# Attention and two expert layers on one core: what releases the loads of q, k and v

## The reference, cut to what matters

```python
scores = scale * np.matmul(q_c, k_c.transpose(0, 1, 2, 4, 3))   # chunks of 64
attn = softmax(scores)                                          # row max taken off, 1e-9 in the sum
out = np.matmul(attn, v_c)
```

## Time and profile before

| | |
|---|---|
| median of 3 runs | 1944.83 us |
| the profiled execution's own time | 1944.43 us |
| its span, first to last instruction | 1942.6 us |
| TensorE busy | 1926.2 us (99%) |
| VectorE, ScalarE, GpSimd busy | 1101.3, 721.2, 520.3 us |
| mean granted clock of TensorE | 1.000 |
| traffic of memory | 61.40 MB, mean 32 GB/s |

### The profile page before, as it was taken

One profiled execution on the slowest core, in us unless ns is written; L12 is line 12 of the kernel. 1 busy time (PEld: TensorE's weight loads), 2 busy tenths in 40 slices (PEclk: granted clock), 3 DMA queues, 4 the chain that ended last, 5 costly groups with the idle time before them and its releaser, 6 DMA issues.

```text
span 1942.6 us, 31606 instructions
## 1 busy us (share of the span) xinstructions
PE 1926.2 (99%) x10756; PEld 1733.7 (89%) x10756; DVE 1101.3 (57%) x1831; ACT 721.2 (37%) x1527; POOL 520.3 (27%) x592
## 2 busy tenths in 40 slices
PE   7999999999999999999999999999999999999999
PEld 6889999999999999999999999999999988888898
DVE  7846655455455555554555555545555586666666
ACT  6632332233223222223232222232332475555554
POOL 6522262222222222222222222222222362222220
PEclk9999999999999999999999999999999999999999
DMA  7100000000000000000000000000000000000002
GB/s 259 70 33 22 22 23 22 22 32 23 31 23 22 22 22 22 22 22 22 22 22 22 22 22 22 22 22 22 22 22 22 22 23 23 22 22 22 22 22 97
DMA packets 19626, 61.40 MB, mean 32 GB/s; under 512 B 2304, under 2 KB 2304, under 8 KB 19584
## 3 DMA queue, kind: packets, MB, share of 16 engines
q1 hardware_dynamic: 19584, 60.84, 9.2%
HBM read 56.12 MB, written 4.72 MB: 31 GB/s over the span
## 4 chain that ended last, share of the span: by engine, by line
PE 98%; DMA 1%; DVE 0%; issue 0%; ACT 0%; SPq 0%; ACTq 0%; DVEq 0%
PE up_banks L598 45%; PE mid_banks L615 4%; PE mid_banks L616 4%; PE mid_banks L628 4%; PE mid_banks L620 4%; PE mid_banks L629 4%; PE mid_banks L630 4%; PE last_banks L628 3%; PE last_banks L620 3%; PE last_banks L616 3%; PE last_banks L615 3%; PE last_banks L629 3%; PE last_banks L630 3%; PE bank L616 1%; PE bank L620 1%; PE bank L615 1%
## 5 line engine op out<-in xcount | busy, mean ns | idle before, releaser
L598 PE MATMUL up_banks<-x_hi,w_hi 128*128 128x384 f32 x1680 | 566.1, 337 | 0.3 <-ACT h_raw L1231 0.3
L598 PE MATMUL up_banks<-x_hi,w_lo 128*128 128x384 f32 x1680 | 564.9, 336 | 0.0
L598 PE MATMUL up_banks<-x_lo,w_hi 128*128 128x384 f32 x1680 | 563.2, 335 | 0.0
L1231 ACT ACTIVATE h_raw<-up_banks 128x384 f32<-128x384 f32 x360 | 176.4, 491 | 727.6 <-PE up_banks L598 717.3
L1654 DVE TENSOR_TENSOR h_raw<-up_banks,h_raw 128x384 f32<-128x384 f32 x360 | 200.4, 557 | 406.0 <-PE up_banks L598 404.2
L414 POOL TENSOR_TENSOR w_sum<-raw 128x256 f32<-128x256 f32 x80 | 59.5, 744 | 1165.9 <-PE up_banks L598 1159.0
L598 PEld LDWEIGHTS up_banks<-x_hi,w_hi 128*128 128x128 f32 x1680 | 315.4, 188 | 10.7 <-ACT h_raw L1231 0.7
L598 PEld LDWEIGHTS up_banks<-x_lo,w_hi 128*128 128x128 f32 x1680 | 315.5, 188 | 5.9
L598 PEld LDWEIGHTS up_banks<-x_hi,w_lo 128*128 128x128 f32 x1680 | 315.2, 188 | 0.0
L1674 DVE SCALAR_TENSOR_TENSOR acc<-mid_banks,route,acc 128x512 f32<-128x512 f32 x252 | 183.7, 750 | 122.2 <-PE mid_banks L630 120.4
L1240 ACT ACTIVATE h_hi<-h_raw 128x384 fp32r<-128x384 f32 x288 | 151.4, 526 | 209.8 <-DVE h_raw L1654 209.8
(11 more groups left out here) (167 smaller groups left out, 2923.9 us busy)
## 6 DMA issues: line engine op xcount, KB each, us to landing
raw<-in_w_up SPq DMA_DIRECT2D x40, 512.0 KB, 3.3
raw<-in_w_down SPq DMA_DIRECT2D x40, 512.0 KB, 3.3
qk<-in_q_k SPq DMA_DIRECT2D x17, 512.0 KB, 4.8
v_rows<-in_v SPq DMA_DIRECT2D x18, 256.0 KB, 3.8
out<-acc SPq DMA_DIRECT2D x18, 256.0 KB, 2.0
qk<-in_q_k SPq DMA_DIRECT2D x2, 256.0 KB, 2.9
gate_raw<-in_w_gate SPq DMA_DIRECT2D x1, 16.0 KB, 3.2
```

The costliest lines, as they stand in the source:

```text
L598: mm = nc.tensor.matmul(up_ps[s], w[:, s, kk, :], xs[:, s, kk, :], start=first and s in (M1, M2, M5), stop=kk == 1 and w is w1_lo, skip_gr ...
L1231: nc.scalar.activation(h_raw[:, to[0], to[1], :], src, ACT.Copy).then_inc(fork_done, 1)
```

## The change

The waits of the second kind are replaced. From the seventh load on (qk 3), a load is issued when the load three places in front of it in the list has landed. The waits inside `load_qk` and `load_v` stay, and so do the order of the loads and everything on the other engines. The small load of the gate weights has no wait of its own and isn't counted. Twenty waits on `scores_done` go, 33 waits on loads come.

```diff
             sp.dma_start(raw2[:, :, :], w_down[0, :, :, :]).then_inc(raw2_loaded, 16)
-            sp.wait_ge(scores_done, 1)
+            sp.wait_ge(raw1_loaded, 16)
             load_qk(3)
-            sp.wait_ge(scores_done, 2)
+            sp.wait_ge(qk_loaded[2], 16)
             load_qk(4)
-            sp.wait_ge(scores_done, 1)
+            sp.wait_ge(raw2_loaded, 16)
             load_v(0)
-            sp.wait_ge(scores_done, 3)
+            sp.wait_ge(qk_loaded[3], 16)
             load_qk(5)
+            sp.wait_ge(qk_loaded[0], 32)
             load_v(2)
+            sp.wait_ge(v_loaded[0], 16)
             load_v(1)
+            sp.wait_ge(qk_loaded[1], 32)
             load_qk(6)
+            sp.wait_ge(v_loaded[2], 16)
             load_qk(7)
-            sp.wait_ge(scores_done, 6)
+            sp.wait_ge(v_loaded[1], 16)
             load_qk(8)
-            sp.wait_ge(scores_done, 4)
+            sp.wait_ge(qk_loaded[2], 32)
             load_v(3)
-            sp.wait_ge(scores_done, 3)
+            sp.wait_ge(qk_loaded[3], 32)
             load_v(5)
+            sp.wait_ge(qk_loaded[0], 48)
             load_qk(9)
+            sp.wait_ge(v_loaded[3], 16)
             load_v(6)
             sp.dma_start(gate_raw[:, :, :], w_gate).then_inc(gate_loaded, 16)
-            sp.wait_ge(scores_done, 6)
+            sp.wait_ge(v_loaded[1], 32)
             load_v(4)
+            sp.wait_ge(qk_loaded[1], 48)
             load_qk(10)
-            sp.wait_ge(scores_done, 5)
+            sp.wait_ge(v_loaded[2], 32)
             load_v(7)
+            sp.wait_ge(v_loaded[0], 32)
             load_v(8)
-            sp.wait_ge(scores_done, 9)
+            sp.wait_ge(qk_loaded[2], 48)
             load_qk(11)
+            sp.wait_ge(v_loaded[3], 32)
             load_qk(12)
...
-            sp.wait_ge(scores_done, 12)
+            sp.wait_ge(v_loaded[2], 48)
             load_v(13)
-            sp.wait_ge(scores_done, 14)
+            sp.wait_ge(v_loaded[1], 48)
             load_qk(14)
-            sp.wait_ge(scores_done, 10)
+            sp.wait_ge(qk_loaded[1], 64)
             load_v(11)
-            sp.wait_ge(scores_done, 13)
+            sp.wait_ge(v_loaded[1], 64)
             load_qk(15)
-            sp.wait_ge(scores_done, 12)
+            sp.wait_ge(qk_loaded[2], 64)
             load_v(12)
-            sp.wait_ge(scores_done, 15)
+            sp.wait_ge(v_loaded[3], 48)
             load_v(14)
-            sp.wait_ge(scores_done, 14)
+            sp.wait_ge(qk_loaded[3], 64)
             load_qk(16)
...
```

More of the change, by code:

```diff
@@ L347, in _ @@
             load_v(8)
-            sp.wait_ge(scores_done, 9)
+            sp.wait_ge(qk_loaded[2], 48)
             load_qk(11)
+            sp.wait_ge(v_loaded[3], 32)
             load_qk(12)
+            sp.wait_ge(v_loaded[0], 48)
             load_v(10)
-            sp.wait_ge(scores_done, 7)
+            sp.wait_ge(qk_loaded[3], 48)
             load_v(9)
-            sp.wait_ge(scores_done, 12)
+            sp.wait_ge(qk_loaded[0], 64)
             load_qk(13)
-            sp.wait_ge(scores_done, 12)
+            sp.wait_ge(v_loaded[2], 48)
@@ L367, in _ @@
             load_v(14)
-            sp.wait_ge(scores_done, 14)
+            sp.wait_ge(qk_loaded[3], 64)
             load_qk(16)
+            sp.wait_ge(v_loaded[0], 64)
             load_v(15)
+            sp.wait_ge(v_loaded[2], 64)
             load_qk(17)
-            sp.wait_ge(scores_done, 16)
+            sp.wait_ge(qk_loaded[0], 80)
             load_v(17)
+            sp.wait_ge(v_loaded[3], 64)
             load_v(16)
```

## The result

The changed kernel takes 1950.24 us, the median of 8 runs (1948.98 to 1951.25). The kernel before, run again beside it, takes 1944.47 (8 runs, 1941.88 to 1950.13). The ratio is 1.0027, interval 1.0018 to 1.0035: slower by 5.8 us, clear of noise and outside the forecast range of 1943.2 to 1947.2. The profiled execution took 1950.17 us with a span of 1948.4, against 1944.43 and 1942.6 before, so the two profiles show the whole difference.

What follows compares the result with a forecast made beforehand. TensorE, busy 1926.2 of 1942.6 us, was taken to bound the kernel. Terms 0 + 0 - 0.1 + 0.2 = +0.1 us gave 1944.5 profiled, median forecast 1944.9 us, no change, range 1943.2 to 1947.2.

Steps and rivals of the forecast that it cites:

- the loop of three loads: Rival: three loads in flight are too few, first seen at tile 4's scores; 3.3 us slower, 1948.2 us, chance 0.15.
- Part A: qk 3 to qk 7: issued later, but landings stay; cost 0, bounds -0.3 to +1.3 us.
- 2.2 is below 2.8: Loads at 5 to 10 us: fixed 2.2 us hidden behind 2.8 us of work from two loads in flight; cost 0.
- Part B: qk 8 to qk 9, about 15 to 25 us: loads go out earlier, nothing gained; 0, bounds -1.4 to +1.4 us.
- Part C: v 6 to qk 12, 25 to 36 us: buffer holds v 6 and loads behind; -0.1 us, from -1.0 to +0.4.
- Part D: v 13 to v 12, 44 to 52 us: qk 15 and v 12 issued later, mostly hidden; +0.2 us, up to 1.6 late.
- The clock: TensorE's slow matmuls until about 25 us: counted as nothing; a shift of their end priced at 2 us either way, chance 0.07.
- last rival: Matmuls get fast at another time than about 25 us; 4 us shift gives 2 us either way, chance 0.07.
- That all arises before 60 us and is carried whole: TensorE has no slack from 60 us on, so any delay or gain there carries one for one to the end.
- the first rival: Three loads in flight too few: +1.3, +0.4 and +1.6 us in three parts of the list, together 3.3; chance 0.15.
- The estimate of 3.2 us for a load of qk: Skill page's time to landing for qk loads; measured shortest 3.6 us was used instead; by the page the sum would be -0.1.

Runs made afterwards that it cites:

- loads: Loads alone, no compute, each released by the landing two to eight places in front; 512 KB at three: 315 GB/s, at six 390.
- early: Changed kernel's waits only on qk 3 to qk 7, the kernel before's waits elsewhere; 1948.17 us, ratio 1.0020 to before.
- mid: Changed kernel's waits only from qk 8 to qk 13, the kernel before's waits elsewhere; 1945.68 us, ratio 1.0007 to before.
- late: Changed kernel's waits only from v 13 on, the kernel before's waits elsewhere; 1947.23 us, ratio 1.0011 to before.
- the two single waits: only15 and only12, each the kernel before with one wait of the changed kernel; ratios 1.0001 and 0.9999 to before.
- depth2: Changed kernel with each load waiting for the landing two places in front instead of three; 1956.53 us, ratio 1.0065 to before.
- gates: Changed kernel with no waits between the loads, only buffers hold a load back; 1944.13 us, ratio 1.0002 to before.
- depth4: Changed kernel with each load waiting for the landing four places in front instead of three; 1946.48 us, ratio 1.0014 to before.
- depth6: Changed kernel with each load waiting for the landing six places in front instead of three; 1945.15 us, ratio 1.0002 to before.
- reorder: Kernel before with v 4, qk 10 ahead of v 6, four loads ahead of v 13, ten `scores_done` waits gone; 1945.70 us, ratio 1.0007.
- only15: Kernel before with only qk 15's wait taken from the changed kernel; 1945.36 us, ratio 1.0001 to before.
- only12: Kernel before with only v 12's wait taken from the changed kernel; 1945.30 us, ratio 0.9999 to before.
- qk34: Kernel before with only the waits of qk 3 and qk 4 taken from the changed kernel; 1947.80 us, ratio 1.0009 to before.

## Why the prediction was wrong

The mechanism that I put second, the loop of three loads, is the one that happened. It had a chance of 0.15 and a price of 3.3 us.

*Part A, taken as 0, bounds -0.3 to +1.3.* This is the step that failed: "2.2 is below 2.8, so the engines don't run dry and the landings stay". qk 3 kept its time (issued at 9.16, landed at 12.96; 12.8 before). qk 4 was issued at 10.40 and took 4.9 us, landing at 15.3, which is the upper bound of the text. qk 5 went out at 12.98, took 6.1, and landed at 19.1, where 16.1 would have kept the old pace; I had set no bound for it at all, since I stopped at tile 4. (6.1 us is a little more than any load took with three in flight in loads, 5.8; what held it isn't shown.) early puts the part at 3.9 us (its interval 2.1 to 5.6). Two things were wrong in the step. I took the load's bytes as served one load after another, so that two loads in flight are 2.8 us of cover; by loads, a load of 512 KB takes 3.9 to 4.7 us to land with only one other in flight and 4.2 to 5.8 with two others, and the engines are busy for 0.89 of the time in a loop of three. And I took the share of 0.94 as a property of the stretch, while it was a property of the waits that the change removed: with qk 3 held until 9.16 the same window shows 0.83.

*Part B, 0.* The cost can't be told from 0, but the mechanism was wrong: qk 8 did not go out at 17.5 but at 20.39, later than before's 20.14, and qk 9 at 26.14 instead of 22.90. Nothing moved earlier, because the loop had already lost that much. mid, which has the waits of parts B and C behind before's start, is +1.4 us with an interval from -0.4 to +3.1.

*Part C, -0.1.* This is the second step that failed: "v 6 is held by its buffer [...] so none of them moves". In after that buffer was free at 24.91, when the values of tile 2 (24.22, 0.69 us) were done, a little earlier than before's. Yet v 6 went out at 27.44, when v 3 had landed (22.89 + 4.5), and v 4 at 28.34, when v 5 had (24.88 + 3.3). The loop held them, and the values of tile 4, which start when v 4 has landed, were 3.0 us late. TensorE itself was 2.0 us late by then (tile 8 at 29.27 against 27.31), behind the hole of 1.75 us; without that hole v 4 would have held it all the same. In mid, where the loads before qk 8 are not in the loop, v 4 lands at 28.7 and nothing of this is seen. So it is part A's lateness that the loop passed on; the text put no wait there.

*Part D, +0.2, upper end 1.6.* late says +2.1 us (0.4 to 3.9), and in neither of the two single waits can a loss be measured. In the profile of after, v 13 to v 12 went as the upper end has it: qk 15 was issued 3.25 us behind v 13, at its landing, and TensorE waited 0.54 us for it and 0.47 for v 12. The sign was right, the size too small.

*The clock, counted as nothing and priced as an independent chance of 0.07.* It isn't independent. In the profile of after, TensorE stood still for 1.26 us before 23.01, for 1.75 before 27.17 and 0.32 before 29.27, and the granted clock fell to the lower level until about 35 us; before has no such spell. Over all runs the mean granted clock falls as the loop gets shorter, from 0.9994 without waits to 0.9970 at two places, and from 0.9991 to 0.9979 from before to after. What that costs is an estimate only. A thousandth of the span is 1.9 us, so 0.0012 is 2.3 us. By the 87 runs of before, in which those at 0.998 took 1946.0 us and those at 1.000 took 1943.1, it is 1.7, but a run that waits longer may also get less clock, so this isn't a measure of the clock alone. And the record of the clock misses a part: it reads 1.00 in the first 25 us of before, where 32 matmuls take 1.13 us. In after the first group of 0.69 us is at 19.23, nearly 6 us earlier than in before. That was the text's own sign for its last rival, on the fast side, and it gave back in this profile about what the later spell cost: TensorE's busy time in all is 0.7 us longer. So in this pair the slower matmuls themselves are worth 0.7 of the 5.8 us; what they cost on the mean of the runs isn't shown. The text's sum of the first and the last rival, 3.3 + 2 = 5.3, comes near the 5.8 by luck: the two terms are not what its parts measured.

*That all arises before 60 us and is carried whole* was right, to 0.3 us: the values of tile 12 are 5.5 late and the span 5.8.

*The range* was built around the value 0 of part A, and the added cases didn't add to each other. The waits along one chain do. It was also said to take in half of the first rival; it takes in 2.3 of its 3.3 us.

*The estimate of 3.2 us for a load of qk.* The Trainium skill (DMA: Bandwidth & Descriptors, "Anatomy of one DMA") gives its formula for transfers that GpSimd issues; the loads of this kernel are issued by SyncE. Two loads of depth2, issued at 10.46 and 24.67, did take 3.2 us. No term of the forecast hung on it.

Left open: what sets the length of the holes named "issue" inside a run of 32 matmuls without a wait. They were 0.3 to 3.5 us long in the profiles, and 0.41 us at most in gates; depth2 has none. They stand at fixed places of the program: before, mid, late, depth4, depth6, reorder, only15 and only12 have one ahead of the last 12 score matmuls of tile 5, and after, early, depth4, gates and qk34 one ahead of the last 22 of tile 7. That speaks for TensorE's instructions as what is missing, but no run tests it, and the length neither grew nor shrank with the number of places (1.75 us at three, up to 1.96 at four and 2.15 at six). Whether a release by the slowest engine or the fixed part of a load is the larger share of the loop's cost is open as well; a wait for fewer than all 16 counts of a load would separate them, and was not tried.

## What to carry to other kernels

A load that is released by the landing of another turns a queue into a loop, and the loop's rate is loads in flight over the time to landing under load, not over the shortest one: with 512 KB a load and about 4.8 us to land, three in flight gave 315 GB/s, and six 390 (loads of 256 KB: 240 and 323). A busy share read in the trace of before says nothing of a stretch whose queue the change takes away. The same holds for what held a load back in before: once the load in front is late, the new wait can take over from the buffer. And when all bounds are on one chain, add them, with the clock as the last term, before a range is set.

## What the runs showed of the hardware

- Time to landing of 512 KB on one queue, in the run loads, behind the first few of each stage: 3.9 to 4.7 us with two in flight, 4.2 to 5.8 with three, 5.0 to 6.1 with four, 7.7 with six; rate 243, 315, 377, 390 GB/s, and 388 with eight.
- Loads of 256 KB: 240 GB/s with three in flight, 277 with four, 323 with six. At the same bytes in flight (six of 256 KB, three of 512 KB) the rates are alike, 323 and 315.
- In the profile of after, the granted clock fell to 0.50 for some 7 us after stops of 1.26, 1.75 and 0.32 us with short matmuls between them.
- With the same loads in the same order, the first 45 us vary by 2 to 3.5 us from one profile to the next (before, late, only15); 87 runs of before lie between 1941.7 and 1948.0 us.
